# Splitting expert weights by quarters, scatters to spare rows of their own, and products of zeros in five waits of TensorE

## What is computed

```
y[t] = r[t] . (state + u*k[t] v[t]);  state = w[t]*state + k[t] v[t]      (per batch and head)

logits = x @ w_gate + modality_bias[modality_id];  e = argmax(logits)
x1 = softmax(logits)[e] * (relu(x @ w1[e]) @ w2[e])

noisy = x1 @ w_gate + log1p(exp(x1 @ w_noise)) * noise;  a, b = top2(noisy)
out = sum over e in (a, b) of weight[e] * (relu(x1 @ w1[e]) @ w2[e])
```

## Time and profile before

| | |
|---|---|
| median of 3 runs | 1000.42 us (1000.36 to 1000.91) |
| profiled execution | 1001.47 us, span 999.8 us |
| mean granted clock | 0.958 |
| PE busy | 910.0 us (91%) |
| DVE busy | 540.0 us (54%) |
| POOL busy | 350.7 us (35%) |
| ACT busy | 228.8 us (23%) |
| chain that ended last | PE 85%, DVE 10% |

### The profile page before, as it was taken

The page is one execution under the profiler, slowest core; times in us unless marked ns, Lnnn a source line. Parts: engine busy times, 40 slices in busy tenths (PEclk is TensorE's granted clock), DMA queues, the critical chain, the costliest instruction groups (busy, mean ns, idle before and its releaser), DMA issues.

```text
span 999.8 us, 22055 instructions
## 1 busy us (share of the span) xinstructions
PE 910.0 (91%) x7285; PEld 881.0 (88%) x7286; DVE 540.0 (54%) x950; ACT 228.8 (23%) x417; POOL 350.7 (35%) x364
## 2 busy tenths in 40 slices
PE   5999999999999999681499999999999999999994
PEld 5888888899999999571499899998998999999894
DVE  8888998784333343249753444435436354543532
ACT  2232333112110121154121312213113131311210
POOL 7333334324322223103434343433534343343232
PEclk9999998999999999795599999999999999999998
DMA  6676782129111102451263444424424444422232
GB/s 246 203 233 217 267 279 78 54 60 360 49 49 40 55 32 64 123 182 47 52 211 56 106 104 115 100 52 108 110 40 102 118 102 114 106 48 42 39 55 42
DMA packets 54447, 111.46 MB, mean 111 GB/s; under 512 B 8688, under 2 KB 35568, under 8 KB 54384
## 3 DMA queue, kind: packets, MB, share of 16 engines
q1 hardware_dynamic: 34752, 71.07, 21.4%
q0 software_dynamic: 15744, 34.70, 17.2%
q10 hardware_dynamic: 3888, 4.89, 1.3%
HBM read 84.84 MB, written 25.81 MB: 111 GB/s over the span
## 4 chain that ended last, share of the span: by engine, by line
PE 85%; DVE 10%; issue 2%; DMA 2%; ACT 0%; DVEq 0%; POOL 0%; POOLq 0%
PE ps L1640 22%; PE ps L1642 22%; PE ps L1641 22%; PE ps L1550 3%; PE ps L1510 2%; PE ps L1514 2%; PE ps L1479 2%; PE ps L1456 2%; DVE weights L1089 2%; PE ps L1541 2%; PE ps L1504 1%; PE ps L1565 1%; PE ps L1577 1%; DVE grow L893 1%; PE ps L1464 1%
## 5 line engine op out<-in xcount | busy, mean ns | idle before, releaser
L1640 PE MATMUL ps<-x_hi,weights 128*128 128x256 f32 x984 | 280.1, 285 | 12.3 <-DVE x_lo L1361 12.3
L1642 PE MATMUL ps<-x_hi,weights 128*128 128x256 f32 x984 | 279.2, 284 | 0.0
L1641 PE MATMUL ps<-x_lo,weights 128*128 128x256 f32 x984 | 279.1, 284 | 0.0
L822 ACT ACTIVATE hid_hi<-ps 128x512 fp32r<-128x512 f32 x164 | 98.3, 599 | 567.3 <-PE ps L1642 567.3
L1640 PE MATMUL ps<-weights,hid_hi 128*128 (+1 forms) x616 | 214.2, 348 | 1.4 <-DVE hid_lo L1366 1.1
L1366 DVE SCALAR_TENSOR_TENSOR hid_lo<-ps,hid_hi 128x512 fp32r<-128x512 f32 x164 | 112.7, 689 | 184.4 <-ACT hid_hi L822 184.4
L1642 PE MATMUL ps<-weights,hid_lo 128*128 (+1 forms) x616 | 207.3, 337 | 0.0
L1641 PE MATMUL ps<-weights,hid_hi 128*128 (+1 forms) x616 | 207.2, 336 | 0.0
L1640 PEld LDWEIGHTS ps<-x_hi,weights 128*128 128x128 f32 x984 | 188.2, 191 | 14.4 <-DVE x_lo L1361 11.4
L1641 PEld LDWEIGHTS ps<-x_lo,weights 128*128 128x128 f32 x984 | 188.4, 191 | 0.0
L1642 PEld LDWEIGHTS ps<-x_hi,weights 128*128 128x128 f32 x984 | 188.2, 191 | 0.0
(11 more groups left out here) (279 smaller groups left out, 1076.8 us busy)
## 6 DMA issues: line engine op xcount, KB each, us to landing
stage<-in_moe_w_dram SPq DMA_DIRECT2D x18, 1536.0 KB, 7.4
kv_in<-in_kv_T_dram SPq DMA_DIRECT2D x24, 512.0 KB, 5.6
kv_in<-in_kv_T_dram SPq DMA_DIRECT2D x24, 448.0 KB, 3.5
w_in<-in_w_T_dram SPq DMA_DIRECT2D x24, 258.5 KB, 4.2
out_dram<-zeros SPq DMA_DIRECT2D x25, 192.0 KB, 8.5
x_rows<-y_tok ACTq DMA_DIRECT2D x24, 192.0 KB, 4.7
stage<-moe_rows SPq DMA_DIRECT2D x12, 384.0 KB, 5.0
stage<-in_moe_w_dram SPq DMA_DIRECT2D x2, 768.0 KB, 7.7
```

What stands on the lines that cost most here:

```text
L822: act.activation(hid_hi[:, 2 * q:2 * q + 2, :], h_ps[q], ACT.Relu).then_inc(s_hhi[l], 1)
L1640: pe.matmul(out_ps, hi, by_hi, start=first, stop=False)
L1641: pe.matmul(out_ps, hi, by_lo, start=False, stop=False)
L1642: return pe.matmul(out_ps, lo, by_hi, start=False, stop=final)
```

## The change

- **w1 by quarters.** ACT and DVE split the next w1 in four quarters, each of the columns of one quarter of the hidden layer, and each as soon as that quarter of the slot is done (`split_w1`, `low_w1`, `w1_quarter`). `up` waits for its own quarter only. In DVE's `slot_step` the first half of the next x (`split_x(..., 0)`) now stands behind the last hid_lo in slots of this kind. The first expert of layer one keeps its halves under new names (`first_w1`, `first_low_w1`).
- **Refill before layer two.** POOL's `split_w2(0)` moves from ahead of the first gather to behind the third. DVE's low part of w1 is half done ahead of the tables and half behind the first `split_x`; `low_w2(1, 0)` moves behind `slot_tables(1)`.
- **Spare rows.** Empty places of tile t get rows of their own for each t, so the output is 128 rows longer and SP clears one block more. The second scatter of a slot in layer two no longer waits for the first, and the first of a slot waits for both of the slot before.
- **Products of zeros.** `keep_busy(n, at)` multiplies the identity with 384 columns of zeros n times, in F32, into PSUM bank `at`: 4 at the start, 13 before the gate stage, 10 before the wait for the choice, 16 behind the counting products, 9 behind the code products.

Left out of the diff below are the size of `spare_row[1]` and its iota (now [P, TS]), the counts of cleared blocks (G + TS in place of G + 1), the renamed calls in the attention stage, and the 128 rows more of the output.

```diff
...
@@ -226,6 +226,10 @@
         w1_raw, w2_raw = stage[:, 0:WSZ], stage[:, WSZ:2 * WSZ]
+        def w1_quarter(tile, at, q):
+            return tile[:, at:at + WSZ].rearrange("p (c f) -> p c f", c=CC)[:, :, q * F // 4:(q + 1) * F // 4]
@@ -475,7 +479,7 @@
                     load_w2(l, e)
-                    sp.wait_ge(s_w1lo[l], n * 2)
+                    sp.wait_ge(s_w1lo[l], n * 4)
...
@@ -638,7 +642,6 @@
                 if l == 1:
-                    split_w2(0)
@@ -656,7 +659,8 @@
                     if l == 1 and not (isinstance(s, int) and s == 0):
-                        pool.wait_ge(s_scatter[l][1 - u][TS - 1], j * 16 + u * 16)
+                        for t in range(TS):
+                            pool.wait_ge(s_scatter[l][1 - u][t], j * 16 + u * 16)
@@ -670,9 +674,6 @@
                         else:
-                            if t > 0:
-                                pool.wait_ge(s_scatter[l][u][t - 1], j * 16 + 16)
-                                pool.nop(nofuse=True)
...
@@ -691,6 +692,7 @@
                 else:
+                    split_w2(0)
...
@@ -763,11 +765,16 @@
-            def split_w1(l, n, a):
-                act.wait_ge(s_w1[l], loaded(l, n, a))
+            def first_w1(a):
+                act.wait_ge(s_w1[0], 16 * (a + 1))
                 act.activation(weights[:, W1_HI + a * HALF:W1_HI + (a + 1) * HALF], w1_raw[:, a * HALF:(a + 1) * HALF],
-                               ACT.Copy).then_inc(s_w1hi[l], 1)
+                               ACT.Copy).then_inc(s_w1hi[0], 2)
+            def split_w1(l, n, q):
+                act.wait_ge(s_w1[l], loaded(l, n, 1))
+                act.activation(w1_quarter(weights, W1_HI, q), w1_quarter(w1_raw, 0, q), ACT.Copy).then_inc(s_w1hi[l], 1)
@@ -834,13 +841,11 @@
                     change, fresh = lookup(act, w1_now[l], s, 1), lookup(act, w2_now[l], s, 1)
-                    for q in range(1, 4):
-                        hidden_high(s, q)
-                    with act.If(change > 0):
-                        act.wait_ge(s_h[l], s * 4 + 4)
-                        act.nop(nofuse=True)
-                        for a in range(2):
-                            split_w1(l, run + 1, a)
+                    for q in range(4):
+                        if q:
+                            hidden_high(s, q)
+                        with act.If(change > 0):
+                            split_w1(l, run + 1, q)
@@ -850,8 +855,8 @@
                     row_hot(0)
-                    for a in range(2):
-                        split_w1(1, 0, a)
+                    for q in range(4):
+                        split_w1(1, 0, q)
...
@@ -1082,13 +1087,19 @@
-            def low_w1(l, n, a):
+            def first_low_w1(a):
...
                 part = slice(a * HALF, (a + 1) * HALF)
-                dve.wait_ge(s_w1hi[l], n * 2 + a + 1)
+                dve.wait_ge(s_w1hi[0], 2 * a + 2)
...
                                   weights[:, W1_HI + a * HALF:W1_HI + (a + 1) * HALF], ALU.subtract)\
-                   .then_inc(s_w1lo[l], 1)
+                   .then_inc(s_w1lo[0], 2)
+            def low_w1(l, n, q):
+                dve.wait_ge(s_w1hi[l], n * 4 + q + 1)
+                dve.tensor_tensor(w1_quarter(weights, W1_LO, q), w1_quarter(w1_raw, 0, q),
+                                  w1_quarter(weights, W1_HI, q), ALU.subtract).then_inc(s_w1lo[l], 1)
@@ -1321,8 +1332,8 @@
                     dve.tensor_tensor(mix[:, :, 1], mix[:, :, 0], exp2[:, :], ALU.mult).then_inc(s_mix, 1)
-                    low_w1(1, 0, 0)
-                    low_w1(1, 0, 1)
+                    for q in range(2):
+                        low_w1(1, 0, q)
@@ -1337,7 +1348,9 @@
                        .then_inc(s_table[l], 1)
-                    link(dve.tensor_scalar(idx_tmp[:, 0:NSl], empty[:, 0:NSl], spare_row[l][:, 0:1], None, ALU.mult))
+                    link(dve.tensor_tensor(idx_tmp[:, 0:NSl].rearrange("p (s t) -> p s t", t=TS),
+                                           empty[:, 0:NSl].rearrange("p (s t) -> p s t", t=TS),
+                                           spare_row[l][:, :].unsqueeze(1).to_broadcast([P, NSX[l], TS]), ALU.mult))
@@ -1390,26 +1403,33 @@
                     split_x(0, 0, 1)
+                    for q in range(2, 4):
+                        low_w1(1, 0, q)
+                    slot_tables(1)
                     low_w2(1, 0)
-                    slot_tables(1)
...
                     hidden_low(s, 0)
-                    hidden_low(s, 1)
...
                         change, fresh = lookup(dve, w1_now[l], s, 1), lookup(dve, w2_now[l], s, 1)
-                    hidden_low(s, 2)
-                    split_x(s + 1, 1 - u, 0)
-                    hidden_low(s, 3)
+                        for q in range(4):
+                            if q:
+                                hidden_low(s, q)
+                            if q == 3:
+                                split_x(s + 1, 1 - u, 0)
+                            with dve.If(change > 0):
+                                low_w1(l, run + 1, q)
+                    else:
+                        hidden_low(s, 1)
+                        hidden_low(s, 2)
+                        split_x(s + 1, 1 - u, 0)
+                        hidden_low(s, 3)
                     if runs_from(l, s):
-                        with dve.If(change > 0):
-                            for a in range(2):
-                                low_w1(l, run + 1, a)
@@ -1442,6 +1462,13 @@
             pe.wait_ge(s_const, 3)
+            def keep_busy(n, at):
+                for _ in range(n):
+                    pe.matmul(ps[:, at, 0:C], ident[:, :], zeros[:, :], start=True, stop=True)
+            keep_busy(4, 5)
@@ -1589,6 +1616,7 @@
                 if l == 1:
+                    keep_busy(13, 4)
@@ -1600,11 +1628,13 @@
                 if l == 1:
+                    keep_busy(10, 7)
...
                       .then_inc(s_count[1], 1)
+                    keep_busy(16, 7)
@@ -1628,6 +1658,7 @@
                     code_products()
+                    keep_busy(9, 7)
@@ -1643,7 +1674,7 @@
-                    pe.wait_ge(s_w1lo[l], run * 2 + 2)
+                    pe.wait_ge(s_w1lo[l], 4 if l == 0 and isinstance(s, int) and s == 0 else run * 4 + q + 1)
...
```

More of the change, by code:

```diff
@@ L84, in attention_moe_moe @@
         iota_s_row_b, iota_row_b = sb("iota_s_row_b", [P, NTX[1]], BF16), sb("iota_row_b", [P, P], BF16)
-        spare_row = [sb("spare_row0", [P, NTX[0]]), sb("spare_row1", [P, 1])]
+        spare_row = [sb("spare_row0", [P, NTX[0]]), sb("spare_row1", [P, TS])]
         zeros = sb("zeros", [P, C])
@@ L487, in _ @@
                             load_run(n, lookup(sp, run_expert, n, E - 1))
-                    for g in range(G + 1):
+                    for g in range(G + TS):
                         clear(g)
@@ L519, in _ @@
                     (tile_row, [[P, G]], 0, 0), (spare_row[0], [[P, NTX[0]]], N, 1),
-                    (spare_row[1], [[1, 1]], N, 1),
+                    (spare_row[1], [[P, TS]], N, 1),
                     (early_tile, [[P, ET]], N, 1), (row_1, [[1, 1]], 1, 1), (tile_no, [[1, 2 * G]], 0, 0)):
@@ L685, in _ @@
                     pool.wait_ge(s_mixst, 16)
-                    pool.wait_ge(s_zero, 16 * (G + 1))
+                    pool.wait_ge(s_zero, 16 * (G + TS))
                     gather(0, 0, 0)
@@ L746, in attention_step @@
                 if late(b, c) in (6, 7):
-                    split_w1(0, 0, late(b, c) - 6)
+                    first_w1(late(b, c) - 6)
                 if late(b, c) in (8, 9):
@@ L955, in attention_step @@
                 if n_late == 10:
-                    low_w1(0, 0, 0)
+                    first_low_w1(0)
                 bonus_values(b, c)
                 if n_late == 10:
-                    low_w1(0, 0, 1)
+                    first_low_w1(1)
                 dve.wait_ge(s_y, 2 + g + 1)
@@ L1770 @@
         args.append(nc.dram_tensor(f"in_{name}_dram", a.shape, _mybir.dt.from_np(a.dtype), kind="ExternalInput").ap())
-    args.append(nc.dram_tensor("out_0_dram", (B * S + 128, H * D), _mybir.dt.float32, kind="ExternalOutput").ap())
+    args.append(nc.dram_tensor("out_0_dram", (B * S + 256, H * D), _mybir.dt.float32, kind="ExternalOutput").ap())
     attention_moe_moe(nc, HP, D, *args)
```

## The result

The changed kernel takes 994.93 us (median of 5, 992.85 to 995.12) where the kernel before took 1000.42 on the same chip: a ratio of 0.9938, with a 95% interval of [0.9924, 0.9953]. The forecast was 979.0, with a range of 973 to 989. Faster was right; the size was not: 5.5 us instead of 21.4. The profiled execution, 992.85 us with a span of 991.1, is the shortest of the five, so the trace shows a gain of 8.6 us and the median 3 less.

A forecast was written before the change was run, and what follows sets the result against it. TensorE was 85% of the chain, so time was to be had only where PE stands or runs at half clock. 9.7 + 4.5 + 2.1 + 3.15 - 1.2 + 3.2 = 21.45 us off 1001.47 gives 980.0, median 979.0; range 973 to 989.

The forecast's parts named there:

- the thirteen take 9.1 us and stand in a wait of 9.79: Before the gate stage: thirteen products of zeros fit in PE's wait for the load of moe_rows and delay nothing.
- The price of a product: One F32 product of zeros with 384 columns takes 0.7 us at full clock and 1.4 at half.
- Rival (c): Products of zeros don't hold the clock up, so their excess is paid and the kernel slows to 1008; chance 0.05.
- Short slots and the clock behind them: Layer two's four short slots: 8.2 us from shorter PE waits, 4.5 from full clock after three of them.
- the relief per slot: An expert's last, short slot in layer two: the next slot starts 2.05 us earlier, bounds 1.0 and 2.4.
- Slot 0: Layer two's first slot: slot tables meet POOL's moved split, giving a new 1.2 us wait for hid_lo, bounds 0 and 3.5.
- the table lookups between them: Slot 0 of layer two: lookups between DVE's first two hid_lo move the second's end from 504.3 to 504.6.
- the refill: Before layer two: mix is stored and the first gather starts 3.15 us earlier, bounds 2 and 3.3.
- the end (3.2): Last scatter of layer two no longer waits for the one before and starts 3.2 us earlier, bounds 1.5 and 3.3.
- the gate stage at a higher clock: Gate stage's first part, at half clock before, gains 1.3 us from the products of zeros, bounds 0 and 2.15.
- the first transposes: Three transposes of layer two's first gather take 0.90 us, a later three 0.49; higher clock gains 0.4.
- Layer one's change of expert: Layer one's one PE wait for x_lo at a change of expert, 1.69 us long, should gain 1.5.

The follow-up runs named there:

- refill_only: The kernel before with only POOL's first split of w2 behind the third gather and low_w2(1, 0) behind the slot tables: 995.89 us, ratio 0.9971.
- spare_only: The kernel before with only the spare rows and without the wait between a slot's two scatters: 994.56 us, ratio 0.9950.
- after_again: The changed kernel once more, unchanged, timed on the third chip: 994.71 us, ratio 0.9959 to the kernel before.
- no_start: The changed kernel without the four products of zeros at the start, the thirteen kept: 994.72 us, ratio 0.9956 to the kernel before.
- one_gate: The changed kernel with one product of zeros instead of thirteen before the gate stage: 989.32 us, ratio 0.9894 to the kernel before.
- products_only: The kernel before with the products of zeros at the same five places and nothing else: 1006.77 us, ratio 1.0071.
- best_three: best1 with the ten, sixteen and nine products of zeros of the gate stage put back: 983.91 us, ratio 0.9851 to the kernel before.
- best1: no_products with DVE's slot tables and loop ends of layer two ahead of the first split_x: 983.82 us, ratio 0.9845 to the kernel before.
- no_products: The changed kernel without any of the five calls for products of zeros: 988.37 us, ratio 0.9895 to the kernel before.

## Why the prediction was wrong, and where it was right

**The step that failed: "the thirteen take 9.1 us and stand in a wait of 9.79".** The price of a product was right: two records at 0.64 us each at half clock and 0.32 at full clock, 1.28 and 0.64 against 1.4 and 0.7. That the wait could be filled was not. A bracket says how long PE stood and what came last. It doesn't say that PE could have worked from its start. It could only after 6.1 us, with 3.7 to 4.4 left, and by then the clock was down, so that the thirteen took 11.3 us and not 9.1. 7.70 instead of 0: of the 12.75 us between forecast and profiled execution (21.45 - 8.7) this is 60%. Rival (c), that products of zeros don't hold the clock, is not what happened: they raised it from 0.50 to 1.00 while they ran.

**Short slots and the clock behind them: 8.2 + 4.5 forecast.** The last line of the table gives -12.85, less 3.2 at the end 9.65 instead of 12.7. Of these, 5.4 are PE standing less (8.2 forecast) and the other 4.3 are left for the clock (4.5 forecast). The clock part was right, also by the windows: 1.00 from 564 to 566 us where it was 0.55, and 1.00 up to 572. The step that was mis-sized is the relief per slot. In the first slot the first wait came as forecast, 2.21 us after hid_hi (2.26 forecast). The slot itself gives 1.02 instead of 2.1 (the others stand for 1.3 to 1.4 less), by two errors. One is arithmetic: transposes that wait until 558.7, turn for 0.48, and 2.35 us of products end at 561.5, not "about 561.2". The other is the 0.78 with "issue" ahead of the next slot, which nothing in the forecast had; it is 0.29 to 0.41 in the others. That PE's own branches or look-ups stand there, hidden before by the 2.05 for x_lo, is argued from their place only.

**Slot 0: 1.2 forecast, 1.43 in the profiled execution, 2.19 to 2.60 in others.** The mechanism was right, POOL's split on the slot tables, and so was the order. That 1.43 lies closer to it than the others do is luck: DVE came later by what the sum had too small, and PE came later too, by its first products at the lower clock. The term that was too small was "the table lookups between them": 0.3 us, where hid_lo's first and second are 1.37 apart. Besides, the higher clock at the first transposes didn't carry over: slot 0's first products take 10.87 us up to the next transposes, before 9.89, because the clock fell behind them instead of ahead of them. The 1.43, these 0.98 and 0.25 between the transposes and the first down product make the line 2.66.

**Right:** the refill (3.13 for 3.15, with the landing of the store as the floor, which came up to 1 us sooner in other executions), the end (3.2), the gate stage at a higher clock (1.07 for 1.3), the first transposes (0.35 for 0.4), four new waits of about 0.6, and that the waits for x_lo would go. Layer one's change of expert gave 0.95 for 1.5; in the six other executions with this edit and no low clock within layer one it is 1.0 to 1.2 (228.6 to 228.8 us against 229.8 in before, refill_only and spare_only). That the start gives 0.1, as forecast, can't be told from these runs.

**The median.** 3 of the 16 us missed lie in no step: the profiled execution of before was 1.05 over its median, that of after 2.1 under it. Nor does this kernel tell 2 us from no change in a single run, as the prediction had it: the 17 times of the kernel before on the third chip lie between 994.83 and 1001.46.

## What to carry to other kernels

An idle time in the trace is room for filler only if the engine can start there: put one cheap instruction in first, and see when it starts, before you fill the rest. After a loop's end that start can be most of the wait, and what is filled in behind it comes out as delay. When two parts of a change are each good alone, look for the place where work that one moved meets work that the other moved: here tables and a split, a wait of 2.2 us, cured by moving the tables into DVE's idle time. With the products of zeros left out that gives 983.8 us.

## What the runs showed of the hardware

- PE starts nothing for 6.04 to 6.26 us behind layer one, whether one or thirteen products follow (five profiled executions: after, after_again, no_start, one_gate, products_only).
- Products of zeros hold the granted clock as others do: they begin at 0.50 (1.2 GHz) and end at 1.00 (2.4 GHz), and a record goes from 0.64 to 0.32 us.
- The clock differs between executions early on: 0.53 or 1.00 from 20 to 22 us in kernels that are the same up to there (best_three, best1), which makes 1.4 us at the second chunk. The low stretch can also move: before it lies in the waits and first products of slot 0 (0.50 to 0.52 from 490 to 496 us), in the changed kernel, with nine products in the wait, some 2 us later (0.50 to 0.59 from 494 to 500), further into slot 0's products.
- Two accumulating scatters into different rows start 1.92 us apart, and the span ends 7.2 us after the last one's start, 7.1 where it had waited for the other to land.
- One of two instructions that meet, DVE's with two SBUF tiles and POOL's, stands for the rest of the other: a DVE operation of 0.18 to 0.45 us took 3.33 to 3.88 beside POOL's split of w2 (before, after, no_products, refill_only), and POOL's split 4.17 instead of 3.5 beside DVE's w2_lo (best1).
